# A fused attention, MLP and routed-expert kernel: a common x2 tile and two common areas, first expert fetched in the first phase, the next three behind the first gather

## The chip, the cores and the metric

The kernel runs on one core of one Trainium2 chip. TensorE is called PE here, VectorE DVE, ScalarE ACT, GpSimd POOL and SyncE SP. SP computes nothing and issues most transfers. The metric is the time of one execution on the device, in microseconds. Lower is better.

## The reference, cut to what matters

Three layers follow each other. A gated linear recurrence over 768 positions for 4 x 8 heads of 48 channels gives 3072 rows of 384 channels (x). An MLP (384 to 2048 to 384, a leaky ReLU with a learned slope) turns x into x2. Then each row is either left alone or sent to one of 8 experts:

```
skip_score = x @ w_skip
do_compute = skip_score > 0
out = x.copy()
xc = x[do_compute]
logits = xc @ w_gate
e_idx = np.argmax(logits, axis=1)
gate_w = probs[np.arange(len(xc)), e_idx]
for e in range(E):
    mask = e_idx == e
    h = np.maximum(xc[mask] @ w1[e], 0.0)
    y[mask] = gate_w[mask, None] * (h @ w2[e])
out[do_compute] = xc + y
```

Here x is the x2 of the MLP. w1 is 8 x 384 x 1024 and w2 is 8 x 1024 x 384, both float32: 1.5 MB each for one expert.

## The kernel before

The program has two phases, each a block of five hand-written instruction streams, one for each engine. Semaphores alone order them. A block ends when all five engines have come to a barrier, and the next begins there.

**Phase 1** handles the rows in eight halves of 384 rows. `step(h)` couples the attention of half h with the MLP of half h-1, so there are eight attention steps, of which seven carry an MLP, and behind the last (h = 7, the last coupled step) stands one MLP pass alone. In a step SP (`step` inside `block.sync`) goes through three chunks c of 128 rows: it loads q, k and v of the next chunk (`load_qkv`), moves decayed q and k from `qk_dec` to `kq` (`move_qk`), moves the attention's output to `xT` (`move_y`, line 359), moves the state (`move_state`, line 367), and at c = 1 calls a function `ahead`, which loads gates for a later half and does nothing in the last coupled step. At the end of each MLP, ACT copies the result from PSUM to the tile `x2` (line 687) and SP stores it twice: to `out` (line 378), as the value of rows that no expert gets, and to `x2_rows` (line 379), a scratch tensor in HBM from which phase 2 gathers. The last instruction of SP in phase 1 waits for the last of these stores.

**Phase 2** has three parts.
- *Routing.* DVE turns the logits, which lie in SBUF, into a table of slots: a slot is a group of up to 128 rows for one expert. PE multiplies the table together with matmuls (line 1274). At the end DVE copies the first slot's row numbers to `gather_at`.
- *The expert slots.* POOL gathers a slot's rows from `x2_rows` into `x_in` (line 1595, an indirect DMA). PE turns them (`turn_x`, line 1280), ACT copies the turned rows from PSUM to `xT_e` (`place_x`, line 1343), PE runs the up matmuls (line 1303), ACT and DVE make the two parts of `hT` (lines 1375, 1544), PE runs the down matmuls (line 1317), DVE adds and POOL scatters to `out` (line 1599). The next slot's gather is issued when the rows of the one before are turned and kept.
- *The expert weights.* There are four buffers for w1 (`w1_v`) and for w2 (`w2_raw`), used by experts p and p + 4. SP's `load(i, p)` issues w1 (line 1248) and w2 (line 1251) of expert 4i + p. ACT splits w2 into a high part (`split`, line 1349) and DVE into a low part (line 1514), so that PE can multiply them at its faster float format with little loss. SP issues experts 0, 1 and 2 at once, and expert 3 when the table is full, because the table's tiles lie in its buffers. Expert 4 is issued when two experts are done, and so on.

ACT's program at the beginning of phase 2, word for word:

```
            split(0, 0)
            split(0, 1)
            place_x(1)
```

After the first slot of expert p (in its program, behind the next slot's `place_x`) ACT splits expert p + 2.

Of the kernel before, what the change touches and what calls it, by code (L numbers as in the profile page):

```python
# [8 lines left out]
ALU = mybir.AluOpType  # L9
# [3 lines left out]
P = 128  # L13
BATCH, HEADS, SEQ, D = 4, 8, 768, 48
DM = HEADS * D
KT = DM // P
TOKENS = BATCH * SEQ
CH = 128
NC = 3
HT = NC * CH  # L20
HALVES = TOKENS // HT
# [9 lines left out]
FE = 1024  # L31
NFE = FE // P
LANES = EXPERTS + 1
GATE_COLS = LANES + 1
DL = DM + GATE_COLS
SLOTROWS = (TOKENS // P + EXPERTS + 1) * P
NOWHERE = 1 << 20
BODY = 4
# [47 lines left out]
def val(count):  # L86

    return count.value() if isinstance(count, Count) else count
# [24 lines left out]
def build(nc, qk, v, a, mask_in, w_in, w_pack, alpha, w_skip, w_gate, w1, w2, out, x2_rows):  # L113
    with ExitStack() as ctx:
        def sem(name):
            return ctx.enter_context(nc.semaphore(name))

        def sb(name, shape, dt=F32):
            return ctx.enter_context(nc.sbuf_tensor(name, shape, dt))

        mlp_ps = [ctx.enter_context(nc.psum_tensor(f"mlp_ps{i}", [P, 512], F32)) for i in range(2)]
        out_ps = [ctx.enter_context(nc.psum_tensor(f"out_ps{i}", [P, 512], F32)) for i in range(3)]
        att_ps = [ctx.enter_context(nc.psum_tensor(f"att_ps{i}", [P, 512], F32)) for i in range(3)]

        ident = sb("ident", [P, P])
        logits = sb("logits", [P, NT, LANES])

        phase1(nc, qk, v, a, mask_in, w_in, w_pack, alpha, w_skip, w_gate, out, x2_rows,
               mlp_ps, out_ps, att_ps, ident, logits)
        phase2(nc, w1, w2, out, x2_rows, mlp_ps, out_ps, att_ps, ident, logits)  # L130


def phase1(nc, qk, v, a, mask_in, w_in, w_pack, alpha, w_skip, w_gate, out, x2_rows,
           mlp_ps, out_ps, att_ps, ident, logits):
    with ExitStack() as ctx:
        def sem(name):
            return ctx.enter_context(nc.semaphore(name))

        def sb(name, shape, dt=F32):
            return ctx.enter_context(nc.sbuf_tensor(name, shape, dt))  # L140
# [8 lines left out]
        slope_side = sb("slope_side", [P, NF])  # L149
        tiny = sb("tiny", [P, 1])  # L150

        gates = [sb(f"gates{i}", [P, 2, NC * DM]) for i in range(2)]
        sq = sb("sq", [P, 2, NC * DM])
        norms = sb("norms", [P, NC * DM])
        inv = sb("inv", [P, NC * DM])
        f_packed = sb("f_packed", [P, KT, NC, 2])
        f_pair = sb("f_pair", [ROWS, 2, PAIRS, NC, 2])

        qk_raw = sb("qk_raw", [P, 2, KT, 2, CH])
        qk_dec = sb("qk_dec", [P, 2, KT, 2, CH])  # L160
        kq = sb("kq", [ROWS, HEADS, 2, CH])
        v_nat = sb("v_nat", [P, 2, DM])
# [10 lines left out]
        bent = sb("bent", [P, 2, HT])  # L173
        g = sb("g", [P, 3, HT])
        g_parts = sb("g_parts", [P, 4, 2, HT], F32R)
        x2 = sb("x2", [P, NC, DL])


        spare = gates[1][:, :, :].rearrange("p r x -> p (r x)")
# [46 lines left out]
        qk_loaded = [sem(f"qk_loaded{i}") for i in range(2)]  # L226
        v_loaded = [sem(f"v_loaded{i}") for i in range(2)]
        k_scaled = sem("k_scaled")
        qk_made = sem("qk_made")
# [14 lines left out]
        g_lo = sem("g_lo")  # L244
        g_used = sem("g_used")
        x2_taken = sem("x2_taken")
        x2_stored = sem("x2_stored")


        def att(h, name, c):  # L250

# [43 lines left out]
        def _(sp):  # L295
# [20 lines left out]
            def load_qkv(h, c):  # L316
                m, _ = buffer_of(h, c)
                n = chunk_no(h, c).value()
                if not isinstance(n, int):
                    sp.reg_mov(chunk_at, n)  # L320
                    n = sp.snap(chunk_at, min_val=0, max_val=HALVES * NC - 1)
                if back(h, c) and back(*back(h, c)):

                    sp.wait_ge(*filled_by("kv", back(*back(h, c))))
                if isinstance(n, int):
                    q_src, v_src = qk[n, :, :], v[n, :, :]
                else:
                    q_src = qk[bass.ds(n, 1), :, :].rearrange("n p x -> (n p) x")
                    v_src = v[bass.ds(n, 1), :, :].rearrange("n p x -> (n p) x")
                sp.dma_start(qk_raw[:, m, :, :, :].rearrange("p t w s -> p (t w s)"), q_src).then_inc(qk_loaded[m], 16)  # L330
                sp.dma_start(v_nat[:, m, :], v_src).then_inc(v_loaded[m], 16)

            def move_qk(h, c):
# [47 lines left out]
            def step(h, mlp_too, more, ahead):  # L381
                for c in range(NC):
                    if c + 1 < NC:
                        load_qkv(h, c + 1)
                        move_qk(h, c + 1)
                    elif more:
                        load_qkv(h.plus(1), 0)
                    move_y(h, c)
                    move_state(h, c)
                    if c == 1:  # L390
                        ahead()
                if more:
                    move_factors(h.plus(1))
                    move_qk(h.plus(1), 0)
                if mlp_too:
                    store_x2(h.plus(-1))
# [33 lines left out]
            with sp.Fori(0, 3) as i:  # L430
# [5 lines left out]
                    sp.nop()  # L436

                step(Half(i, 2), True, True, load_but_last)
            step(Half(0, HALVES - 1), True, False, lambda: None)
            store_x2(Half(0, HALVES - 1))  # L440
            sp.wait_ge(x2_stored, val(32 * HALVES + 1))


        @block.tensor
# [337 lines left out]
        def _(dve):  # L782
# [89 lines left out]
            def decay_qk(h, c):  # L872

                g_ = chunk_no(h, c)
                m, loads = buffer_of(h, c)
                dve.wait_ge(qk_loaded[m], loads)
                dve.wait_ge(f_inverted, val(g_ + 1))
                k_ = qk_raw[:, m, :, 1, :]
                dve.tensor_tensor(k_, k_, tiles(of_chunk(inv[:, :], c)), ALU.mult).then_inc(k_scaled, 1)
                if back(h, c):  # L880
                    dve.wait_ge(qk_moved, val(g_ * (32 * len(OP_MOVES))))
                dve.wait_ge(k_scaled, val(g_ + 1))
                for r in range(2):
                    G = tiles(of_chunk(gates[h.p][:, r, :], c)).unsqueeze(2).broadcast_to([P, KT, 2, CH])
                    last = dve.tensor_tensor(qk_dec[:, r, :, :, :], qk_raw[:, m, :, :, :], G, ALU.mult)
                last.then_inc(qk_made, 1)

            def mask_scores(h, c):
# [217 lines left out]
                               pattern=[[-1, P]], channel_multiplier=1).then_inc(consts, 1)  # L1106


def phase2(nc, w1, w2, out, x2_rows, mlp_ps, out_ps, att_ps, ident, logits):
    with ExitStack() as ctx:  # L1110
        def sem(name):
            return ctx.enter_context(nc.semaphore(name))

        def sb(name, shape, dt=F32):
            return ctx.enter_context(nc.sbuf_tensor(name, shape, dt))


        w1_v = [sb(f"w1_sb{p}", [P, KT, FE]) for p in range(BODY)]
        w2_raw = [sb(f"w2_raw{p}", [P, NFE, DM]) for p in range(BODY)]
        w2_v = [[sb(f"w2_{part}{p}", [P, NFE, DM], F32R) for part in ("hi", "lo")] for p in range(BODY)]  # L1120
        BIG = float(NOWHERE)
        NJ = NT
# [43 lines left out]
        in_row = w1_v[BODY - 1][:, :, :].rearrange("p k (t x) -> p (k t) x", x=P)  # L1166
        gather_at = sb("gather_at", [P, 1], I32)
        scatter_at = sb("scatter_at", [P, 1], I32)
        x_in = sb("x_in", [P, DM])
        x_kept_rows = sb("x_kept_rows", [P, 2, DM])  # L1170
        xT = sb("xT_e", [P, KT, P])
        hT = sb("hT", [P, 2, NFE, P], F32R)
        y = sb("y", [P, DM])

        step = sem("step")
        exp_made = sem("exp_made")
# [12 lines left out]
        tab_made = sem("tab_made")  # L1189
        first_at = sem("first_at")  # L1190
        pads_made = sem("pads_made")
        w1_loaded = [sem(f"w1_loaded{p}") for p in range(BODY)]
        w2_loaded = [sem(f"w2_loaded{p}") for p in range(BODY)]
        w2_hi = sem("w2_hi")
        w2_lo = sem("w2_lo")
        expert_done = sem("expert_done")
# [44 lines left out]
        @block.sync  # L1241
        def _(sp):
            def load(i, p):
                if i > 0:

                    sp.wait_ge(expert_done, i * BODY + p - (BODY - 3))
                    sp.wait_ge(w1_loaded[p], 16 * i)
                sp.dma_start(w1_v[p][:, :, :], expert(w1, i, p).rearrange("e (k p) f -> p (e k) f", p=P)).then_inc(w1_loaded[p], 16)  # L1248
                if i > 0:
                    sp.wait_ge(w2_lo, i * BODY + p - (BODY - 1))  # L1250
                sp.dma_start(w2_raw[p][:, :, :],
                             expert(w2, i, p).rearrange("e (f p) d -> p (e f) d", p=P)).then_inc(w2_loaded[p], 16)

            for p in range(BODY - 1):
                load(0, p)
            sp.wait_ge(table_full, 1)
            load(0, BODY - 1)
            for i in range(1, EXPERTS // BODY):
                for p in range(BODY):
                    load(i, p)  # L1260
# [315 lines left out]
        def _(pool):  # L1576
# [12 lines left out]
            pool.affine_select(out=before_pp[:, :], in_=before_pp[:, :], compare_op=ALU.is_gt, fill=0.0, base=0,  # L1589
                               pattern=[[1, P]], channel_multiplier=-1).then_inc(triangles, 1)  # L1590
            pool.memset(x_in[:, :], 0.0).then_inc(pads_made, 1)
            pool.memset(y[:, :], 0.0).then_inc(pads_made, 1)

            def gather():
                pool.indirect_dma_start(x_in[:, :], None, x2_rows, bass.IndirectOffsetOnAxis(ap=gather_at[:, 0:1], axis=0),
                                        bounds_check=TOKENS - 1, oob_is_err=False).then_inc(x_gathered, 16)
# [2 lines left out]
                pool.indirect_dma_start(out, bass.IndirectOffsetOnAxis(ap=scatter_at[:, 0:1], axis=0), y[:, :], None,  # L1599
                                        bounds_check=TOKENS - 1, oob_is_err=False).then_inc(y_stored, 16)  # L1600

            pool.wait_ge(pads_made, 2)
            pool.wait_ge(first_at, 2)
            gather()
            pool.wait_ge(slots_known, 1)
            slots_all = pool.value_load(slots_i[0:1, EXPERTS:EXPERTS + 1], min_val=0, max_val=NSLOT - 2)
            turned, kept, made = (pool.alloc_register(x) for x in ("turned", "kept", "made"))
# [92 lines left out]
```

## Time and profile before

| | |
|---|---|
| time, median of 3 runs | 968.17 us (966.34 to 971.03) |
| profiled execution | 968.83 us, span 966.9 us |
| mean granted TensorE clock | 0.922 of full speed |
| PE, DVE, ACT busy | 751.7, 699.2, 367.4 us |
| POOL busy | 51.8 us |
| loads of w1, w2 in phase 2 | 8 of 1536 KB each |
| end of phase 1 to first expert matmul | 761.6 to 805.1 us |
| expert slots | 805.1 to the end |

The span is the time from the first to the last instruction of the profiled execution. The granted clock is a share of TensorE's full speed; 1.0 stands for 2.4 GHz and 0.5 for 1.2 GHz. "Landing" is the time from the issue of a transfer to its semaphore's signal. A name such as SPq stands for an engine's sequencer, which issues transfers, waits and branches. Times in the rows count from the span's start.

### The profile page before, as it was taken

What the parts mean: (1) busy time and instruction counts of PE and PEld (TensorE: products, weight loads), DVE (VectorE), ACT (ScalarE), POOL (GpSimd) and SP (SyncE); (2) the same over time, 40 slices, a digit from 0 to 9 for tenths busy, and PEclk for the clock granted to TensorE, in tenths of its full rate; (3) what the DMA queues carried; (4) which work ended last, traced back from release to release, by engine and by line L of the source; (5) the groups of instructions that cost most, each with busy time, mean ns of one, the idle gap of its engine ahead of it and who ended that gap; (6) DMA issues with size and microseconds to landing.
All of it is one profiled execution on the core that took longest, in us unless ns stands there. A gap on an engine that the chain in (4) does not pass through costs nothing. (4 is left out here: it accounts for less than half of the span.)

```text
span 966.9 us, 16131 instructions
## 1 busy us (share of the span) xinstructions
PE 751.7 (78%) x5478; PEld 723.3 (75%) x5479; DVE 699.2 (72%) x1231; ACT 367.4 (38%) x805; POOL 51.8 (5%) x48
## 2 busy tenths in 40 slices
PE   1343456987897989889798889979999547998786
PEld 1333456987886989788688788879999447998786
DVE  6967988988999799898899989875333373434333
ACT  5452234435434534433453353334433222322221
POOL 1000000000000000000000000000000012233122
PEclk9999567999999899999999999999999857999799
DMA  6542343243342424424242352233210393324520
GB/s 188 178 152 79 93 118 90 64 130 113 80 109 62 139 65 115 126 66 133 70 118 73 100 151 63 70 113 97 57 56 1 133 357 110 126 73 163 205 82 17
DMA packets 82433, 104.74 MB, mean 108 GB/s; under 512 B 15990, under 2 KB 68384, under 8 KB 82336
## 3 DMA queue, kind: packets, MB, share of 16 engines
q1 hardware_dynamic: 80544, 99.69, 35.2%
q0 software_dynamic: 1792, 3.76, 1.2%
q8 instruction: 61, 1.00, 0.4%
q14 instruction: 36, 0.29, 0.1%
HBM read 61.04 MB, written 12.19 MB: 76 GB/s over the span
## 5 line engine op out<-in xcount | busy, mean ns | idle before, releaser
L524 PE MATMUL out_ps<-w_out_hi,g_parts 128*128 128x394 f32 x768 | 225.3, 350 | 26.3 <-DVE g_parts L933 26.3
L514 PE MATMUL mlp_ps<-xT,w_in_hi 128*128 128x384 f32 x768 | 207.1, 351 | 20.3 <-DMA xT<-y_parts 8.6
L524 PEld LDWEIGHTS out_ps<-w_out_hi,g_parts 128*128 128x128 f32 x768 | 145.9, 193 | 30.3 <-DVE g_parts L933 30.2
L514 PEld LDWEIGHTS mlp_ps<-xT,w_in_hi 128*128 128x128 f32 x768 | 140.5, 194 | 27.5 <-issue 13.5
L928 DVE SCALAR_TENSOR_TENSOR g<-mlp_ps,slope_side,bent 128x384 f32<-128x384 f32 x128 | 78.6, 615 | 83.4 <-ACT bent L666 75.3
L524 PE MATMUL out_ps<-w_out_lo,g_parts 128*128 128x394 f32 x384 | 133.8, 348 | 0.0
L514 PE MATMUL mlp_ps<-xT,w_in_lo 128*128 128x384 f32 x384 | 131.2, 342 | 0.0
L666 ACT ACTIVATE bent<-mlp_ps,bend_size 128x384 f32<-128x384 f32 x128 | 73.7, 576 | 149.5 <-PE mlp_ps L514 149.0
L1303 PE MATMUL mlp_ps<-xT_e,w_sb 128*128 128x128 f32 x624 | 79.5, 290 | 19.3 <-issue 14.1
L1303 PEld LDWEIGHTS mlp_ps<-xT_e,w_sb 128*128 128x128 f32 x624 | 77.4, 205 | 22.1 <-issue 16.9
L672 ACT ACTIVATE g_parts<-g 128x384 fp32r<-128x384 f32 x128 | 66.2, 517 | 35.4 <-DVE g L928 35.4
L468 PE MATMUL att_ps<-ident,kq 112*128 112x112 f32 x192 | 27.5, 295 | 60.8 <-DMA kq<-qk_dec 60.8
L1544 DVE SCALAR_TENSOR_TENSOR hT<-mlp_ps,hT 128x256 fp32r<-128x256 f32 x52 | 21.8, 424 | 72.8 <-ACT hT L1375 72.8
L524 PEld LDWEIGHTS out_ps<-w_out_lo,g_parts 128*128 128x128 f32 x384 | 74.1, 193 | 0.0
L514 PEld LDWEIGHTS mlp_ps<-xT,w_in_lo 128*128 128x128 f32 x384 | 74.1, 193 | 0.0
L660 ACT ACTIVATE s_t<-s_in,f_pair 112x96 f32<-112x96 f32 x192 | 53.6, 362 | 52.9 <-DVE s_in L912 34.1
L468 PEld LDWEIGHTS att_ps<-ident,kq 112*128 112x128 f32 x192 | 22.9, 160 | 65.5 <-DMA kq<-qk_dec 55.2
L933 DVE TENSOR_TENSOR g_parts<-g,g_parts 128x384 fp32r<-128x384 f32 x128 | 70.3, 549 | 0.3
L459 PE MATMUL att_ps<-kq 112*128 112x128 f32 x384 | 60.5, 320 | 5.3 <-ACT k_back L634 5.3
L798 DVE RECIPROCAL sq<-sq 128x384 f32<-128x384 f32 x24 | 61.1, 2547 | 1.2 <-ACT sq L614 1.2
L459 PEld LDWEIGHTS att_ps<-kq 112*128 112x128 f32 x384 | 57.1, 234 | 6.4 <-ACT k_back L634 6.4
L870 DVE RECIPROCAL inv<-norms 128x384 f32<-128x384 f32 x24 | 60.0, 2529 | 0.0
(150 smaller groups left out, 1082.8 us busy)
## 6 DMA issues: line engine op xcount, KB each, us to landing
kq<-qk_dec SPq DMA_DIRECT2D x96, 144.0 KB, 3.0
w_sb<-in_w SPq DMA_DIRECT2D x8, 1536.0 KB, 7.7
w_raw<-in_w SPq DMA_DIRECT2D x8, 1536.0 KB, 12.0
gates<-in_a SPq DMA_DIRECT2D x24, 384.0 KB, 4.3
qk_raw<-in_qk SPq DMA_DIRECT2D x24, 384.0 KB, 4.2
xT<-y_parts SPq DMA_DIRECT2D x48, 144.0 KB, 2.8
v_nat<-in_v SPq DMA_DIRECT2D x24, 192.0 KB, 4.0
out<-x SPq DMA_DIRECT2D x8, 576.0 KB, 3.2
```

The source lines that it names most:

```text
L459: last = pe.matmul(ps[:, n * CH:(n + 1) * CH], kq[:, slot, 1, :], kq[:, slot, 0, :], start=True, stop=True)
L468: last = pe.transpose(ps[:, n * ROWS:(n + 1) * ROWS], kq[:, PAIRS * half + n, 1, :], ident[0:ROWS, 0:ROWS])
L514: last = pe.matmul(ps[:, 0:HT], w_in_v[s][:, kk, f * P:(f + 1) * P], xT[n.p][:, kk, m, :], start=(kk == 0 and j == 0), stop=(kk == KT - 1 ...
L524: last = pe.matmul(out_ps[i][:, 0:DL], g_parts[:, f % 4, s, i * P:(i + 1) * P], w_out_v[m][:, f, :], start=(f == 0 and j == 0), stop=(f == ...
L660: last = act.activation(s_t[:, r, :, pair_, :], s_in[:, :, pair_, :], ACT.Copy, scale=f_pair[:, h.p, pair_, c, r:r + 1])
L666: act.activation(bent[:, f % 2, :], mlp_ps[f % 2][:, 0:HT], ACT.Relu, scale=bend_size[:, f:f + 1]).then_inc(bent_made, 1)
L672: act.activation(g_parts[:, f % 4, 0, :], g[:, f % 3, :], ACT.Copy).then_inc(g_hi, 1)
L798: dve.reciprocal(s1, s0).then_inc(norm_inv, 1)
L870: dve.reciprocal(of_chunk(inv[:, :], c), of_chunk(norms[:, :], c)).then_inc(f_inverted, 1)
L928: dve.scalar_tensor_tensor(out=g[:, f % 3, :], in0=mlp_ps[f % 2][:, 0:HT], scalar=slope_side[:, f:f + 1], in1=bent[:, f % 2, :], op0=ALU.m ...
L933: dve.tensor_tensor(g_parts[:, f % 4, 1, :], g[:, f % 3, :], g_parts[:, f % 4, 0, :].bitcast(F32), ALU.subtract).then_inc(g_lo, 1)
L1303: last = pe.matmul(mlp_ps[g % 2][:, (f % 2) * P:(f % 2 + 1) * P], w1_v[p][:, kk, f * P:(f + 1) * P], xT[:, kk, :], start=(kk == 0), stop=( ...
```

## The change

1. The tile `x2` becomes a part of a tile `rows` that belongs to the whole kernel. `x_in`, `x_kept_rows` and `y` of phase 2 lie in the same tile. The semaphore `x2_stored` belongs to the whole kernel too. SP no longer waits for the last stores at the end of phase 1; POOL waits for them ahead of the first gather. `x_in` lies beside x2's part, so its memset may run early; `y`'s lies in it, and its memset moves behind the first gather.
2. Two areas `arena[0]` and `arena[1]` belong to the whole kernel. In phase 1 each holds one buffer of the gates and one of raw q and k; in phase 2 the first holds w1 and the second w2 of expert 0 (and 4). SP fetches expert 0's weights in the last coupled step, at `ahead`.
3. SP issues experts 1, 2 and 3 when the first gather has landed. The wait for the full table in front of expert 3 goes, since that gather follows the table.

ACT's, PE's and DVE's programs keep their order.

```diff
+        arena = [sb(f"arena{i}", [P, KT * FE]) for i in range(2)]
+        rows = sb("rows", [P, NC * DL + DM])
+        x2_stored = sem("x2_stored")
+        first_loaded = [sem(f"first_loaded{i}") for i in range(2)]
...
-        gates = [sb(f"gates{i}", [P, 2, NC * DM]) for i in range(2)]
+        gates = [arena[i][:, 0:2 * NC * DM].rearrange("p (r x) -> p r x", r=2) for i in range(2)]
...
-        qk_raw = sb("qk_raw", [P, 2, KT, 2, CH])
+        qk_raw = [arena[i][:, 2 * NC * DM:2 * NC * DM + 2 * KT * CH].rearrange("p (t w s) -> p t w s", t=KT, w=2)
+                  for i in range(2)]
...
-        x2 = sb("x2", [P, NC, DL])
+        x2 = rows[:, 0:NC * DL].rearrange("p (i d) -> p i d", i=NC)
...
-            step(Half(0, HALVES - 1), True, False, lambda: None)
+            def fetch_first_expert():
+                sp.wait_ge(qk_made, NC * HALVES)
+                sp.dma_start(arena[0][:, :].rearrange("p (k f) -> p k f", k=KT),
+                             w1[0:1].rearrange("e (k p) f -> p (e k) f", p=P)).then_inc(first_loaded[0], 16)
+                sp.dma_start(arena[1][:, :].rearrange("p (f d) -> p f d", f=NFE),
+                             w2[0:1].rearrange("e (f p) d -> p (e f) d", p=P)).then_inc(first_loaded[1], 16)
+
+            step(Half(0, HALVES - 1), True, False, fetch_first_expert)
             store_x2(Half(0, HALVES - 1))
-            sp.wait_ge(x2_stored, val(32 * HALVES + 1))
...
-        x_in = sb("x_in", [P, DM])
-        x_kept_rows = sb("x_kept_rows", [P, 2, DM])
+        x_in = rows[:, NC * DL:NC * DL + DM]
+        x_kept_rows = rows[:, 0:2 * DM].rearrange("p (a d) -> p a d", a=2)
...
-        y = sb("y", [P, DM])
+        y = rows[:, 2 * DM:3 * DM]
...
-            for p in range(BODY - 1):
+            sp.wait_ge(x_gathered, 16)
+            for p in range(1, BODY):
                 load(0, p)
-            sp.wait_ge(table_full, 1)
-            load(0, BODY - 1)
...
-            pool.memset(y[:, :], 0.0).then_inc(pads_made, 1)
+            pool.wait_ge(x2_stored, 32 * HALVES + 1)
...
-            pool.wait_ge(pads_made, 2)
+            pool.wait_ge(pads_made, 1)
             pool.wait_ge(first_at, 2)
             gather()
+            pool.memset(y[:, :], 0.0).then_inc(pads_made, 1)
```

How SP's program reads before, from the last state moves of phase 1 to expert 3 (w_sb is a w1 buffer, w_raw a w2 buffer, in_w either weight tensor; in brackets what the row waits for):

```order
L367 DMA s_stack<-state 48x192 x3
L378 DMA out<-x 128x3x384 [waits x2_taken]
L379 DMA x_rows<-x 128x3x384
L378 DMA out<-x 128x3x384 [waits x2_taken]
L379 DMA x_rows<-x 128x3x384
L135 UNCONDITIONAL_BRANCH [waits x2_stored]
L1241 UNCONDITIONAL_BRANCH [waits barrier_Pool_Activation_PE_DVE_SP_release]
L1248 DMA w_sb<-in_w 128x3x1024
L1251 DMA w_raw<-in_w 128x8x384
```

How it reads in the changed kernel, from the second chunk's state moves of the last coupled step:

```order
L370 DMA s_stack<-state 48x192 x3
L444 DMA arena<-in_w 128x3x1024 [waits qk_made]
L446 DMA arena<-in_w 128x8x384
L362 DMA xT<-y_parts 48x6x128 [waits att_free1]
L362 DMA xT<-y_parts 48x6x128
```

And from the last stores of phase 1 on:

```order
L381 DMA out<-rows 128x3x384 [waits x2_taken]
L382 DMA x_rows<-rows 128x3x384
L139 UNCONDITIONAL_BRANCH
L1252 UNCONDITIONAL_BRANCH [waits barrier_Pool_Activation_PE_DVE_SP_release]
L1259 DMA w_sb<-in_w 128x3x1024 [waits x_gathered]
L1262 DMA w_raw<-in_w 128x8x384
L1259 DMA w_sb<-in_w 128x3x1024
```

Expert 0's two transfers moved ahead of the last chunk's moves, the wait on `x2_stored` is gone, and the first transfer of phase 2 now waits for `x_gathered`.

ACT in the changed kernel, from the end of phase 1 to its first slot (w_hi is the high part of w2):

```order
L139 UNCONDITIONAL_BRANCH
L1346 UNCONDITIONAL_BRANCH [waits barrier_Pool_Activation_PE_DVE_SP_release]
L1349 ACT_TABLE_LOAD
L1349 ACTIVATE expd<-diff 128x192 [waits diff_made]
L1359 ACTIVATE w_hi<-arena 128x3072 [waits first_loaded1]
L1359 ACTIVATE w_hi<-w_raw 128x3072 [waits w2_loaded1]
L1353 ACTIVATE xT_e<-att_ps 128x384 [waits x_turned]
```

The order is that of before; what moved is only the issue of the transfer that the second split waits for.

## Rows read from the trace of the kernel before

**Rows 1.** Waits of SP's queue: line <- releaser: total us, times, longest us.
```profile
SPq L135 <- DMA x_rows<-x: 3.7, 1, 3.7
...
SPq L135 <- PEq L135: 0.2, 1, 0.2
```

**Rows 2.** Timeline of the seam: start us, us, engine, line, instruction [idle before].
```profile
761.09 0.54 ACT L687 ACTIVATE x<-out_ps 128x384 f32<-128x384 f32 x1
...
762.06 0.49 SPq L379 DMA_DIRECT2D x_rows<-x  x1
...
766.73 0.35 DVE L1402 TENSOR_REDUCE top<-logits 128x24 f32<-128x192 f32 x1 [10.61 <-PEq L135]
```

**Rows 3.** Chain of waits, start us, us, what; first gather to ACT's copy.
```profile
794.48 8.75 DMA x_in<-x_rows,gather_at
...
803.37 0.88 PE att_ps L1280 x3
...
804.28 0.50 ACT xT_e L1343
```

**Rows 4.** Timeline of PE, first slot, turn of the next rows, and slot at 898.
```profile
805.06 7.30 PE L1303 MATMUL mlp_ps<-xT_e,w_sb 128*128 128x128 f32 x48 [0.82 <-ACT xT_e L1343]
...
812.20 0.49 PE L1280 MATMUL att_ps<-ident,x_in 128*128 128x128 f32 x3
...
898.45 8.35 PE L1303 MATMUL mlp_ps<-xT_e,w_sb 128*128 128x128 f32 x48 [6.80 <-issue]
```

**Rows 5.** Timeline of SP and PE, end of the last coupled step.
```profile
683.67 2.97 SPq L367 DMA_DIRECT2D s_stack<-state  x4
...
695.42 4.60 SPq L359 DMA_DIRECT2D xT<-y_parts  x6
...
708.98 0.51 PE L514 MATMUL mlp_ps<-xT,w_in_hi 128*128 128x384 f32 x2
```

**Rows 6.** Timeline of SP and ACT: loads of expert 0, splits of 0 and 1.
```profile
766.68 0.38 SPq L1248 DMA_DIRECT2D w_sb<-in_w  x1
...
767.11 0.48 SPq L1251 DMA_DIRECT2D w_raw<-in_w  x1
...
777.67 2.76 ACT L1349 ACTIVATE w_hi<-w_raw 128x3072 fp32r<-128x3072 f32 x1 [9.32 <-DMA w_raw<-in_w]
...
785.85 2.76 ACT L1349 ACTIVATE w_hi<-w_raw 128x3072 fp32r<-128x3072 f32 x1 [5.42 <-DMA w_raw<-in_w]
```

**Rows 7.** Landing of w2 loads (line 1251) issued at 767.11 and 868.63.
```profile
DMA to landing us min/median/max: 10.5/10.5/10.5
...
DMA to landing us min/median/max: 11.9/11.9/11.9
```

**Rows 8.** Landing of gathers (line 1595) starting 794, 824, 846, 868, 834.
```profile
DMA to landing us min/median/max: 8.8/8.8/8.8
...
DMA to landing us min/median/max: 3.1/3.1/3.1
...
DMA to landing us min/median/max: 5.3/5.3/5.3
...
DMA to landing us min/median/max: 6.2/6.2/6.2
...
DMA to landing us min/median/max: 9.2/9.2/9.2
```

**Rows 9.** Timeline of DVE's subtraction and POOL's first two gathers.
```profile
793.35 3.35 DVE L1514 TENSOR_TENSOR w_lo<-w_raw,w_hi 128x3072 fp32r<-128x3072 f32 x1
...
794.48 3.27 POOL L1595 DMA_INDIRECT x_in<-x_rows,gather_at  x1 [25.14 <-issue]
...
805.13 1.00 POOL L1595 DMA_INDIRECT x_in<-x_rows,gather_at  x1 [7.38 <-PE att_ps L1280]
```

**Rows 10.** Windows: us, busy by engine, granted clock, DMA share, GB/s.
```profile
808.00:809.00 1.00, 1.00 (x8) 1.00 (x8) 0.42 (x1) 0.38 (x1) 0.00 (x0) 0.69 0.03 1
...
904.00:905.00 1.00, 1.00 (x10) 1.00 (x10) 0.42 (x1) 0.35 (x1) 0.00 (x0) 0.91 0.00 0
```

More of the change, by code:

```diff
@@ L126, in build, with phase1 @@
         logits = sb("logits", [P, NT, LANES])
[L128 to L134, printed above, removed]
+        arena = [sb(f"arena{i}", [P, KT * FE]) for i in range(2)]
+        rows = sb("rows", [P, NC * DL + DM])
+        x2_stored = sem("x2_stored")
+        first_loaded = [sem(f"first_loaded{i}") for i in range(2)]
+        phase1(nc, qk, v, a, mask_in, w_in, w_pack, alpha, w_skip, w_gate, w1, w2, out, x2_rows,
+               mlp_ps, out_ps, att_ps, ident, logits, arena, rows, x2_stored, first_loaded)
+        phase2(nc, w1, w2, out, x2_rows, mlp_ps, out_ps, att_ps, ident, logits, arena, rows, x2_stored, first_loaded)
+def phase1(nc, qk, v, a, mask_in, w_in, w_pack, alpha, w_skip, w_gate, w1, w2, out, x2_rows,
+           mlp_ps, out_ps, att_ps, ident, logits, arena, rows, x2_stored, first_loaded):
     with ExitStack() as ctx:
@@ L246, in phase1 @@
         x2_taken = sem("x2_taken")
-        x2_stored = sem("x2_stored")
         def att(h, name, c):
@@ L329, in load_qkv @@
                     v_src = v[bass.ds(n, 1), :, :].rearrange("n p x -> (n p) x")
-                sp.dma_start(qk_raw[:, m, :, :, :].rearrange("p t w s -> p (t w s)"), q_src).then_inc(qk_loaded[m], 16)
+                sp.dma_start(qk_raw[m].rearrange("p t w s -> p (t w s)"), q_src).then_inc(qk_loaded[m], 16)
                 sp.dma_start(v_nat[:, m, :], v_src).then_inc(v_loaded[m], 16)
@@ L877, in decay_qk @@
                 dve.wait_ge(f_inverted, val(g_ + 1))
-                k_ = qk_raw[:, m, :, 1, :]
+                k_ = qk_raw[m][:, :, 1, :]
                 dve.tensor_tensor(k_, k_, tiles(of_chunk(inv[:, :], c)), ALU.mult).then_inc(k_scaled, 1)
@@ L884, in decay_qk @@
                     G = tiles(of_chunk(gates[h.p][:, r, :], c)).unsqueeze(2).broadcast_to([P, KT, 2, CH])
-                    last = dve.tensor_tensor(qk_dec[:, r, :, :, :], qk_raw[:, m, :, :, :], G, ALU.mult)
+                    last = dve.tensor_tensor(qk_dec[:, r, :, :, :], qk_raw[m][:, :, :, :], G, ALU.mult)
                 last.then_inc(qk_made, 1)
@@ L1106, in _, with phase2 @@
                                pattern=[[-1, P]], channel_multiplier=1).then_inc(consts, 1)
-def phase2(nc, w1, w2, out, x2_rows, mlp_ps, out_ps, att_ps, ident, logits):
+def phase2(nc, w1, w2, out, x2_rows, mlp_ps, out_ps, att_ps, ident, logits, arena, rows, x2_stored, first_loaded):
     with ExitStack() as ctx:
@@ L1115, in sb @@
             return ctx.enter_context(nc.sbuf_tensor(name, shape, dt))
-        w1_v = [sb(f"w1_sb{p}", [P, KT, FE]) for p in range(BODY)]
-        w2_raw = [sb(f"w2_raw{p}", [P, NFE, DM]) for p in range(BODY)]
+        w1_v = [arena[0][:, :].rearrange("p (k f) -> p k f", k=KT),
+                *(sb(f"w1_sb{p}", [P, KT, FE]) for p in range(1, BODY))]
+        w2_raw = [arena[1][:, :].rearrange("p (f d) -> p f d", f=NFE),
+                  *(sb(f"w2_raw{p}", [P, NFE, DM]) for p in range(1, BODY))]
         w2_v = [[sb(f"w2_{part}{p}", [P, NFE, DM], F32R) for part in ("hi", "lo")] for p in range(BODY)]
@@ L1191, in phase2 @@
         pads_made = sem("pads_made")
-        w1_loaded = [sem(f"w1_loaded{p}") for p in range(BODY)]
-        w2_loaded = [sem(f"w2_loaded{p}") for p in range(BODY)]
+        w1_loaded = [first_loaded[0], *(sem(f"w1_loaded{p}") for p in range(1, BODY))]
+        w2_loaded = [first_loaded[1], *(sem(f"w2_loaded{p}") for p in range(1, BODY))]
         w2_hi = sem("w2_hi")
```

## The prediction

> **What bounds the kernel now.** I read the waits of the DMA-issuing queue first, because two of the three edits move transfers there. The last rows of the first phase show a wait of 3.7 us at the block's end for the last x2_rows store, and only 0.2 us for the other engines [rows 1]. The timeline of that place gives the same: the last x2 tile is copied by 761.63, both stores are issued by 762.55, and the vector engine's first routing instruction starts at 766.73 [rows 2]. Then the chain of waits: up to the first gather at 794.48 it holds routing on DVE and PE and no transfer, so loads of expert weights bound nothing there. The gather takes 8.75 us; PE turns the rows at 803.37, ACT copies them at 804.28 [rows 3], and the first expert matmul starts at 805.06 [rows 4]. So the path through the seam is: stores, routing, gather, turn, copy, expert 0. The MLP pass before it is PE's alone.
>
> I call the start of the first expert matmul X (805.06 before). Everything behind it is driven by X: slots are chained, and each of the second four experts is loaded when earlier experts are done. So the prediction is the sum of what moves X, and of what the first slots then find.
>
> **Edit 1, no wait at the seam.** The 3.7 us of [rows 1] leave the path. The two stores' issue stays in it, and so does the barrier (762.55 + 3.7 = 766.25, to about 766.7). The wait comes back on POOL ahead of the first gather. It costs nothing there: the stores land about 766.3, and the gather starts 24 us later even after the shift. Were that cover gone, the 3.7 us would be back. Bounds: a gain of 3.7, or 0 if another engine holds the barrier; the 0.2 us row says that the others are there. I take -3.7, so the gather starts at 794.48 - 3.7 = 790.78.
>
> **Edit 2, expert 0 fetched in the last coupled step.** Two 1.5 MB transfers are issued by SP behind the state moves that end at 683.67 + 2.97 = 686.64, ahead of the xT moves at 695.42 [rows 5]. The wait that they carry (all q and k decayed) is met by then, because SP passed the same count before its last kq moves. The matching pair at 766.68 and 767.11 takes 0.9 us of issue [rows 6], and its second part lands 10.5 us after its issue [rows 7], so here about 697.6. The six xT moves behind can be late by 2 to 3 us. They are all issued by 695.42 + 4.60 = 700.0, and the last MLP pass reads them at 708.98 [rows 5]; even with a generous 5 us of flight, 4 us are left for that delay. Cost 0; were the cover gone, those 2 to 3 us would stand on PE's path. Gain 0 as well: expert 0's split was done in the shade of the routing before (ACT at 777.67 [rows 6]). Moving y's memset behind the gather is nothing: POOL is idle on both sides.
>
> **Edit 3, experts 1 to 3 behind the gather.** Two effects of opposite sign.
>
> *The gather alone on the queues.* Before, it ran beside expert 3's load, issued when the table was full, and landed after 8.8 us. Five landings compare [rows 8], in the order of the group: 8.8 for it; 3.1 (the gather at 824.53) and 5.3 (846.66) with no load in the way; 6.2 (868.47) and 9.2 (834.74) with one. The 5.3 us kind is that in which POOL's own part takes 3.2 instead of 1.0 us; it occurs while DVE's long subtraction for a weight split runs. For the first gather that is so in both kernels: DVE issues the subtraction (793.35, 3.35 us) right behind the index copies, POOL's part takes 3.27 and ends 1.05 us after it, while the second gather's takes 1.00 [rows 9]. So I take 5.2 us for 8.75: it lands at 796.0, a gain of 3.55. Bounds: 3.1 and 8.75.
>
> The Trainium skill, SBUF — State Buffer, section "Who interferes with whom", infers that a tensor_tensor on VectorE takes only the read side of the port pair shared with GpSimd and leaves descriptor generation free. By that rule the gather would land after 3.1 us and the sum would be 2.1 us lower. The trace shows 3.27 us of POOL beside exactly such an instruction, so the sum goes by the trace, and the rule's outcome is the third rival.
>
> *The new wait.* ACT runs in order, and in its program the split of expert 1's w2, which waits for that w2, stands ahead of the copy that releases the first matmul. Before, expert 1's w2 was there long ahead of the gather. Now SP issues it only when the gather has landed. Behind the split on ACT stands the copy, and behind the copy PE's whole expert part and DVE's share of it. The same pair of loads on an empty queue, with more queued behind, is in the trace: first issue at 766.68, ACT's split begins at 777.67, that is 10.99 us [rows 6]. Then the split itself, 2.76 us [rows 6], and an estimated 0.1 us for SP to wake (PE's turn follows the landing, 794.48 + 8.75 = 803.23, by 0.14 [rows 3]): 795.98 + 0.1 + 10.99 + 2.76 = 809.83 for the copy. Copy behind landing was 804.28 - 803.23 = 1.05 us and becomes 13.85: a cost of 12.80. From copy to first matmul 0.78 us, as before: X = 810.6. Bounds: 10.5 or 11.9 us of landing for the w2 transfer [rows 7], the latter for +1.4; and 0 for the whole cost if ACT weren't held.
>
> So X moves by -3.7 - 3.55 + 12.80 = **+5.55 us**.
>
> **What the first slots then find.**
> - *Clock.* Before, PE turned x at 803.37, 1.7 us ahead of X, and the granted clock left 0.50 within 808 to 809; the first slot's up matmuls took 7.30 us. At 898.45 PE came out of an idle stretch with nothing ahead of it, the clock rose about 904, and the same matmuls took 8.35 us [rows 4, 10]. In the changed kernel the turn stands 14 us ahead of X, so I take the second row: +1.05. Bounds 0 and 1.05.
> - *Second gather.* It is issued 0.07 us after X [rows 9], and PE wants it at 812.20 [rows 4], 7.14 us after X (8.2 with the slow clock). Experts 1 to 3 are 9.4 MB; at 11 us for the first 3.1 and 8.2 for each further 3.1 (ACT's second split began at 785.85, 8.18 after the first, when its w2 had come [rows 6]) they fill the queues until about 823. DVE is idle then, so it is of the 3.1 us kind, and that takes 6.2 us beside a load. Cost 0, upper bound 9.2 - 7.14 = 2.1.
> - *Experts 2 and 3.* Their w2 lands about 815 and 823. ACT wants the first of them when slot 1's turned rows are copied, 8 us after X, and the other in expert 1's first slot, some 28 us after X. Cost 0.
>
> Sum: 5.55 + 1.05 = **+6.6 us**. The profiled execution has a span of 966.9 and took 968.83 us, 1.9 more; it would be 975.4. The median of the runs is 968.17, 0.66 below the profiled one, so I forecast **974.8 us**.
>
> **Rivals.**
> 1. *The second gather waits for the held-back loads too.* Place: PE's turn in expert 0's first slot. It decides when a gather on full queues takes more than 7.1 to 8.2 us. For: 8.8 and 9.2 were seen. Against: both ran beside DVE's subtraction, the second won't. Price 2.1: 976.9 us.
> 2. *ACT isn't held; the loads are off the path* (the other side). If the gather alone released the copy, only the gains would be left: -3.7 - 3.55 = -7.25, 960.9 us. It decides if expert 1's w2 is there by the time PE has turned x. Against: such a load took over 10 us from its issue [rows 7], its issue waits for that gather, and the order of ACT's rows leaves no way round.
> 3. *The first gather is of the quick kind and the clock comes back as before.* It lands after 3.1, and there is no clock term: 5.55 - 2.1 = +3.45, 971.6 us. For: 3.1 was seen at 824.53. Against: the same DVE instruction still starts 1.1 us ahead of it.
> 4. *The seam's wait isn't lost but moves* to another engine's arrival at the barrier: 6.6 + 3.7, 978.5 us. Against: the 0.2 us row.
>
> **How the numbers follow.** Forecast 0.62, rival 1 0.12, rival 2 0.07, rival 3 0.15, rival 4 0.04. A change under 0.5% (4.8 us) can't be told from none for this kernel. Slower beyond it are the forecast, less 0.03 that comes out just under 4.8, and rivals 1 and 4: 0.75. Within: rival 3 and that 0.03: 0.18. Faster: rival 2, 0.07. The range runs from 970.5 (rival 3 and a little more) to 978.5 (the forecast with 11.9 us of landing and rival 1's price, or rival 4).
>
> **What would show it.** Right: DVE's first routing row comes about 1.4 us after ACT's last x2 copy, not 5.1; the first gather lands about 5.2 us after its start; ACT stands idle for about 39 us ahead of the second weight split, with a w2 transfer as the releaser, and its copy of xT follows that split; the first expert matmul lies about 19.8 us behind the first gather's start, against 10.6 before; from there to the end the distances are those of before within 2 us. Wrong: xT copied ahead of the second split, a gap in PE around 709, or a first gather that stays above 8 us on empty queues.

## The result, and the profile after

The changed kernel takes 974.05 us in the median of 8 runs (972.05 to 976.63); the kernel before, run beside it (8 runs), 968.16. The ratio is 1.0065, with a 95% interval of 1.0046 to 1.0084. The forecast was 974.8 us. The profiled execution has a span of 972.0 us against 966.9, so 5.1 us are to be found in the two traces.

First the waits of SP's queue in the changed kernel (engine line <- releaser: total us, times, longest), which answer to [rows 1]:

```profile
SPq L1259 <- DMA rows<-x_rows,gather_at: 33.2, 1, 33.2
...
SPq L139 <- PEq L139: 0.2, 1, 0.2
```

The row of the stores is gone, and the rest of the barrier is what it was. In its place stands one wait of 33.2 us for the first gather, at the first weight load of phase 2. SP's waiting costs nothing by itself; what is queued behind it does. The timeline of the seam (start us, us, engine, line, instruction, [idle before]), to set against [rows 2]:

```profile
761.98 0.54 ACT L696 ACTIVATE rows<-out_ps 128x384 f32<-128x384 f32 x1
...
762.96 0.49 SPq L382 DMA_DIRECT2D x_rows<-rows  x1
...
763.89 0.35 DVE L1412 TENSOR_REDUCE top<-logits 128x24 f32<-128x192 f32 x1 [6.88 <-PEq L139]
```

From the start of the last x2 copy to DVE's first routing row it was 766.73 - 761.09 = 5.64 us and is 1.91. Then the same view from the first gather on, to set against [rows 3, 4, 6, 9]:

```profile
791.66 3.25 POOL L1605 DMA_INDIRECT rows<-x_rows,gather_at  x1 [25.64 <-issue]
...
797.00 0.38 SPq L1259 DMA_DIRECT2D w_sb<-in_w  x1
...
797.12 0.88 PE L1290 MATMUL att_ps<-ident,rows 128*128 128x128 f32 x3 [7.11 <-DMA rows<-x_rows,gather_at]
...
797.44 0.48 SPq L1262 DMA_DIRECT2D w_raw<-in_w  x1
...
809.34 2.76 ACT L1359 ACTIVATE w_hi<-w_raw 128x3072 fp32r<-128x3072 f32 x1 [41.18 <-DMA w_raw<-in_w]
...
812.01 0.47 ACT L1353 ACTIVATE xT_e<-att_ps 128x384 f32<-128x384 f32 x1
...
812.71 7.29 PE L1313 MATMUL mlp_ps<-xT_e,arena 128*128 128x128 f32 x48 [14.71 <-ACT xT_e L1353]
```

Read it as an order in time: the gather lands, the rows are turned at once, and then PE has nothing to do for 14.7 us, while ACT has stood 41 us in front of one split. Its releaser is the w2 transfer that SP issued at 797.44. The copy of the turned rows is ready to go from 798 on and follows only behind that split.

Stage by stage, in us, from the rows of both traces:

| stage | before | after | difference |
|---|---|---|---|
| start to last x2 copy | 761.09 | 761.98 | +0.89 |
| last x2 copy to first routing row | 5.64 | 1.91 | -3.73 |
| routing, to start of first gather | 27.75 | 27.77 | +0.02 |
| start of gather to turn | 8.89 | 5.46 | -3.43 |
| turn to first expert matmul | 1.69 | 15.59 | +13.90 |
| first expert matmul to the end | 161.84 | 159.29 | -2.55 |
| span | 966.9 | 972.0 | +5.1 |

The first row isn't an effect of the change: SP's state moves, which stand ahead of the new fetch, start 1.0 us later already, and over the ten traces that share this first phase (the changed kernel, e1 and e3 to e10) the last x2 copy starts anywhere from 757.37 to 761.98. The end of the coupled step, to set against [rows 5]:

```profile
684.67 2.95 SPq L370 DMA_DIRECT2D s_stack<-state  x4
687.67 0.58 SPq L444 DMA_DIRECT2D arena<-in_w  x1
688.30 0.49 SPq L446 DMA_DIRECT2D arena<-in_w  x1
696.30 4.61 SPq L362 DMA_DIRECT2D xT<-y_parts  x6
```

The xT moves come 11.63 us after the start of the state moves, where it was 11.75 before, and PE goes from the last coupled matmul to the pass alone without a gap:

```profile
709.69 0.34 PE L533 MATMUL out_ps<-w_out_hi,g_parts 128*128 128x394 f32 x1
709.87 0.51 PE L523 MATMUL mlp_ps<-xT,w_in_hi 128*128 128x384 f32 x2
```

### The profile page after: what moved, and what is told of

It reads as the page before. It is cut to its first block and busy times, and to the rows that moved or that the text cites. A ratio compares the mean times of both kernels' runs of the same rounds, so it can differ in the third digit from the quotient of the medians.

```text
span 972.0 us, 16130 instructions
## 1 busy us (share of the span) xinstructions
PE 754.1 (78%) x5478; PEld 726.3 (75%) x5479; DVE 699.7 (72%) x1231; ACT 367.6 (38%) x805; POOL 51.8 (5%) x48
## 5 line engine op out<-in xcount | busy, mean ns | idle before, releaser
L1313 PE MATMUL mlp_ps<-xT_e,w_sb 128*128 128x128 f32 x480 | 59.6, 286 | 7.5 <-issue 7.1
L1313 PEld LDWEIGHTS mlp_ps<-xT_e,w_sb 128*128 128x128 f32 x480 | 58.2, 201 | 9.3 <-issue 8.4
## 6 DMA issues: line engine op xcount, KB each, us to landing
w_raw<-in_w SPq DMA_DIRECT2D x6, 1536.0 KB, 11.9
```

The costliest lines, as they stand in the source:

```text
L1313: last = pe.matmul(mlp_ps[g % 2][:, (f % 2) * P:(f % 2 + 1) * P], w1_v[p][:, kk, f * P:(f + 1) * P], xT[:, kk, :], start=(kk == 0), stop=( ...
```

## The experiments

The theory is that the whole loss is one coupling: SP issues expert 1's w2 behind the gather, and ACT's program has the split of that w2 ahead of the copy that starts expert 0. The rivals are that the held-back loads cost because they come late for their own slots or crowd the slots' gathers, and that the seam or the fetch costs. The times are medians of 5 to 12 runs, each with its ratio to the kernel before, run beside it, and the 95% interval of that ratio, unless said otherwise. Edits are shown against the changed kernel, cut to what matters.

**e1: expert 1 ahead of the gather.**

```diff
+            load(0, 1)
             sp.wait_ge(x_gathered, 16)
-            for p in range(1, BODY):
+            for p in range(2, BODY):
                 load(0, p)
```

> The changed kernel, with expert 1's load issued at the start of phase 2 and only experts 2 and 3 behind the first gather. Theory (the whole loss is ACT waiting for expert 1's w2 ahead of its copy of the turned rows): the w2 is there 25 us before the gather, the copy follows the turn, first matmul about 1.8 us behind the gather's landing; 13 to 14 us less than the changed kernel, 960.5 to 962, 0.7% below the kernel before. Rival (the held-back loads cost by crowding the slots' gathers and by arriving late for their own experts): experts 2 and 3 are still behind the gather and two of three loads still crowd it, so at most a third is won back, 969 to 972. Rival (the loss is elsewhere, in the coupled step or at the seam): 974, no change.

Measured 960.0 us, ratio to before 0.9935 (0.9908 to 0.9963): 1.3% below the changed kernel by the two ratios. Its timeline:

```profile
790.62 3.24 POOL L1606 DMA_INDIRECT rows<-x_rows,gather_at  x1 [25.64 <-issue]
...
796.07 0.87 PE L1291 MATMUL att_ps<-ident,rows 128*128 128x128 f32 x3 [7.11 <-DMA rows<-x_rows,gather_at]
...
797.70 7.22 PE L1314 MATMUL mlp_ps<-xT_e,arena 128*128 128x128 f32 x48 [0.75 <-ACT xT_e L1354]
```

Turn to first matmul is 1.63 us again. One load moved, two still held, and the whole loss is back: the first rival falls. What the two held loads do cost shows at the third gather (807.17). Expert 3's load is still under way beside it, and PE idles for 0.69 us ahead of the turn of those rows:

```profile
815.53 0.55 PE L1291 MATMUL att_ps<-ident,rows 128*128 128x128 f32 x3 [0.69 <-DMA rows<-x_rows,gather_at]
```

**e4: ACT's order.**

```diff
             split(0, 0)
-            split(0, 1)
             place_x(1)
+            split(0, 1)
```

> The changed kernel with two lines of ACT exchanged: it copies the turned rows ahead of the split of expert 1's w2. All loads stay where the change has them. Theory (the place in ACT's order is what couples the first slot to the load): the first matmul comes about 1.8 us behind the gather's landing, not 15.8, but ACT then stands in the split when the first result is ready, so the first hT comes when w2 has landed and been split, 15 us behind the landing against 19 before; PE has two groups of up matmuls done by then and the clock may have fallen again; 3 to 5 us less than the changed kernel, 969 to 971. Rival (the order on ACT doesn't matter, DVE or PE wait for the loads too): 974.

Measured 970.26 us, ratio 1.0039 (1.0015 to 1.0062), between the kernel before and the changed one. The interval overlaps that of the changed kernel (1.0046 to 1.0084), so the gain over it isn't clear by time alone; the trace carries the reading. The timeline shows the stall where it was forecast, on the other side of the copy:

```profile
793.43 0.49 ACT L1353 ACTIVATE xT_e<-att_ps 128x384 f32<-128x384 f32 x1 [29.88 <-PE att_ps L1290]
794.19 5.01 PE L1313 MATMUL mlp_ps<-xT_e,arena 128*128 128x128 f32 x24 [0.80 <-ACT xT_e L1353]
...
804.52 2.76 ACT L1359 ACTIVATE w_hi<-w_raw 128x3072 fp32r<-128x3072 f32 x1 [10.60 <-DMA w_raw<-in_w]
...
808.06 2.29 PE L1313 MATMUL mlp_ps<-xT_e,arena 128*128 128x128 f32 x9 [8.86 <-DVE hT L1554]
```

PE starts 1.7 us behind its turn (792.52 in that trace), fills both mlp_ps buffers with two groups (24 of 48 matmuls), and waits 8.86 us, because ACT stands at the split, first waiting for its w2 and then in it, and can't take them. The load is as late as before; what it stops is set by ACT's order. With e1 this shows the coupling from both sides.

**e8: w2 ahead of w1.**

```diff
             sp.wait_ge(x_gathered, 16)
-            for p in range(1, BODY):
+            sp.dma_start(w2_raw[1][:, :, :], ...).then_inc(w2_loaded[1], 16)
+            sp.dma_start(w1_v[1][:, :, :], ...).then_inc(w1_loaded[1], 16)
+            for p in range(2, BODY):
                 load(0, p)
```

> The changed kernel, with w2 of expert 1 issued ahead of its w1 behind the gather. Theory (ACT waits for exactly this w2): it lands after 8.0 us, as the first of a pair does, instead of 11.9 after an issue 0.44 later, so the first matmul comes 4.3 us earlier; w1 isn't wanted before expert 0's slots are over. 969.5 to 970, ratio to before 1.002. Rival (ACT waits for the whole pair, or a gather behind full queues is what is late): 974.

Measured 970.01 us, ratio 1.0013 (0.9995 to 1.0031). The awaited transfer and what follows it:

```profile
796.17 0.38 SPq L1266 DMA_DIRECT2D w_raw<-in_w  x1
...
804.72 2.76 ACT L1361 ACTIVATE w_hi<-w_raw 128x3072 fp32r<-128x3072 f32 x1 [37.40 <-DMA w_raw<-in_w]
...
808.09 1.22 PE L1315 MATMUL mlp_ps<-xT_e,arena 128*128 128x128 f32 x4 [10.92 <-ACT xT_e L1355]
```

From the start of the first gather to the first matmul it is 808.09 - 790.83 = 17.26 us, 3.8 less than the 21.05 of the changed kernel (812.71 - 791.66), and the time follows by 0.5%. The forecast was 4.3: ACT's split began 8.55 us after the issue of w2, not 8.0. The time goes with the arrival of exactly this w2.

**e2 and e3: the seam alone; the seam and the fetch.** In e2 the fetch in the coupled step is left out and all loads are where they were before. In e3 the fetch stays:

```diff
-            sp.wait_ge(x_gathered, 16)
-            for p in range(1, BODY):
+            for p in range(1, BODY - 1):
                 load(0, p)
+            sp.wait_ge(table_full, 1)
+            load(0, BODY - 1)
```

> The tiles of the changed kernel, no wait for the last stores at the seam, but all weight loads where they were before (0, 1, 2 at the start of phase 2, 3 with the full table) and none in the coupled step. Theory: only the 3.7 us of the seam are won, the first gather still takes 8.8 us beside expert 3's load; 964.5, ratio to before about 0.996. Rival (the stores' wait comes back elsewhere, or the new placement of tiles costs in phase 1): 968, ratio 1.000. If loads that start 3.7 us earlier beside the stores mattered, the stores would land later, and nothing would wait for them.

> As the run with the seam alone, and expert 0 fetched in the last coupled step; experts 1 and 2 at the start of phase 2, 3 with the full table. Theory: the fetch is worth nothing by itself and costs nothing; 964.5, equal to the run with the seam alone within 0.2%; first gather 8 to 9 us, because expert 3's load still starts with it. Rival (it was the rest of expert 2's load, not expert 3's, that slowed the gather): that rest is gone here, the gather takes 5.3 us and the time is 961. Rival (the fetch delays the xT moves): a gap on PE at 709 and 966 to 967.

Measured 963.79 us, ratio 0.9962 (0.9939 to 0.9984), and 962.95 us, ratio 0.9966 (0.9941 to 0.9991). The seam is worth 3.7 us by the median ratio of e2 (1.5 to 5.9 by its interval), and e2's trace has 761.61 - 759.69 = 1.92 us from the last x2 copy to the first routing row, as the changed kernel has. The fetch is worth nothing that can be measured. The first gather is slow in both. In e3 (starts of the gather and of the first matmul):

```profile
789.99 3.25 POOL L1606 DMA_INDIRECT rows<-x_rows,gather_at  x1 [25.64 <-issue]
...
800.49 0.79 PE L1314 MATMUL mlp_ps<-xT_e,arena 128*128 128x128 f32 x2 [0.75 <-ACT xT_e L1354]
```

That is 10.50 us, as before (10.58). In this trace no transfer ran from 784 to 788, so of the weight loads only expert 3's, issued at 788.36, ran beside the gather: it is that load that slows the gather.

**e5: only expert 3 held.** As e3, with the wait for the gather in place of the wait for the table:

```diff
+            for p in range(1, BODY - 1):
+                load(0, p)
             sp.wait_ge(x_gathered, 16)
-            for p in range(1, BODY):
-                load(0, p)
+            load(0, BODY - 1)
```

> The changed kernel, with experts 1 and 2 loaded at the start of phase 2 and only expert 3 behind the first gather: all three edits kept, the loads held back cut to the one that ran beside that gather before. Theory: seam 3.7 less, first gather 5.3 instead of 8.8 (expert 3's load alone slowed it: the run with the fetch and expert 3 at the full table had 10.5 us from gather to first matmul, as before), nothing waits for a weight in the first slots; 960 to 961, ratio to before 0.992 to 0.993, about 2 us less than the run with seam and fetch. Rival (what the gather wins, the second gather loses, because expert 3's load now falls on it): 963, as the run with seam and fetch.

Measured 960.76 us, ratio 0.9915 (0.9894 to 0.9935). Gather to first matmul is 7.09 us, 3.4 less than in e3:

```profile
788.23 3.25 POOL L1606 DMA_INDIRECT rows<-x_rows,gather_at  x1 [25.64 <-issue]
...
795.32 1.00 PE L1314 MATMUL mlp_ps<-xT_e,arena 128*128 128x128 f32 x3 [0.75 <-ACT xT_e L1354]
```

The held load doesn't delay the second gather enough to show: PE has no idle time ahead of the second turn. The intervals of the two ratios (0.9894 to 0.9935, and 0.9941 to 0.9991 for e3) only just miss each other; the traces set e5 clearly apart.

**e6: DVE's subtraction behind the first gather.** As e5, and:

```diff
-            split(0, 0)
             keep_x(1)
+            split(0, 0)
```

> As the run with only expert 3 held, and DVE keeps the first slot's rows ahead of its subtraction for expert 0, so that the subtraction no longer stands beside POOL's part of the first gather. Theory (the subtraction holds up POOL's descriptor work): POOL's part of the first gather takes 1.0 instead of 3.25 us, it lands after 3.1 instead of 5.3, first matmul about 4.9 us behind the gather's start instead of 7.1, 958 to 959. Rival (the Trainium skill, SBUF — State Buffer, section 'Who interferes with whom': a tensor_tensor leaves descriptor generation free; the 3.25 us are a first use of the path or chance): POOL's part stays at 3.25 and the time at 960.5. A second possibility: the subtraction falls on the second gather and delays that one instead, with a stall of PE ahead of the second turn and no gain.

Measured 957.3 us, ratio 0.9878 (0.9861 to 0.9894): the fastest version here, 1.2% below the kernel before and 1.9% below the changed one. Its interval meets that of e5 at 0.9894, so the gain over e5 rests on the trace, where it is 5.08 us from the start of the gather to the first matmul, and 7.09 in e5.

```profile
791.00 1.18 POOL L1606 DMA_INDIRECT rows<-x_rows,gather_at  x1 [25.64 <-issue]
...
794.39 0.87 PE L1291 MATMUL att_ps<-ident,rows 128*128 128x128 f32 x3 [5.05 <-DMA rows<-x_rows,gather_at]
794.62 3.35 DVE L1525 TENSOR_TENSOR w_lo<-arena,w_hi 128x3072 fp32r<-128x3072 f32 x1
...
796.08 8.39 PE L1314 MATMUL mlp_ps<-xT_e,arena 128*128 128x128 f32 x48 [0.81 <-ACT xT_e L1354]
796.15 2.70 POOL L1606 DMA_INDIRECT rows<-x_rows,gather_at  x1 [3.53 <-PE att_ps L1291]
...
804.82 0.55 PE L1291 MATMUL att_ps<-ident,rows 128*128 128x128 f32 x3 [0.34 <-DMA rows<-x_rows,gather_at]
```

POOL's part of the first gather falls from 3.25 to 1.18 us when the subtraction is gone from beside it, so the 3.25 are no cost of a first use. The second gather's part rises from 1.01 to 2.70, ending 0.88 us behind the subtraction that now stands beside it; PE waits 0.34 us for it, where e5, with expert 3's load beside the second gather too, had no wait. So here a subtraction with both inputs in SBUF does hold up POOL's part of an indirect transfer. The Trainium skill, SBUF — State Buffer, section "Who interferes with whom", infers that a tensor_tensor leaves descriptor generation free; the same section says that such an instruction, with two inputs in SBUF, contends with a GpSimd instruction that reads SBUF, and this gather takes its row numbers from there. The inference fails here; whether the reading of the row numbers is why, no run tells.

**e7, e9, e10: why the awaited w2 took 11.9 us and not 10.5.** In e7 POOL waits for expert 1's w2 ahead of the second gather. In e9 expert 3's weights are read in the place of expert 1's, so expert 1's rows get the wrong ones. In e10 nothing is queued behind the awaited w2:

```diff
 e7
+            pool.wait_ge(w2_loaded[1], 16)
             slots_all = pool.value_load(...)
 e10
             sp.wait_ge(x_gathered, 16)
-            for p in range(1, BODY):
+            load(0, 1)
+            sp.wait_ge(w2_loaded[1], 16)
+            for p in range(2, BODY):
                 load(0, p)
```

> The changed kernel, with POOL waiting for expert 1's w2 before it issues the second gather and the first scatter. In the changed kernel these two ran during that w2's transfer, which landed 11.9 us after its issue, where 10.5 was reckoned. Theory (the two crowd it): landing 10.5 and first matmul 1.4 us earlier, 19.6 us behind the first gather's start instead of 21.05. Rival (three more loads queued behind it, or HBM, make the difference): 11.9 again. No stall at the second turn is expected, since the second gather then has 7 us beside 1.4 us of split and copy, and takes 6.4.

> The changed kernel; where expert 1's weights are loaded, expert 3's are read instead, so expert 1's rows are computed with the wrong weights. Question: why the w2 behind the gather took 11.9 us from its issue in the changed kernel and 10.5 for expert 0 (10.6 for expert 3) before. If where the weights lie in HBM decides, this one lands in 10.6 as expert 3's did before, and the first matmul comes 1.3 us earlier. If what runs beside it decides (the gather after, loads queued behind), it stays at 11.7 to 11.9.

> The changed kernel with experts 2 and 3 issued only when expert 1's w2 has landed: nothing is queued behind the awaited transfer. If the loads behind crowd it, it lands in 10.5 us or less; if not, 11.7 to 11.9 again. Expert 2's w2 then lands about 20 us behind expert 1's issue and 8 us later than now, so ACT's split of it (wanted 8 us behind the first matmul) waits some 3 us and the second slot with it; time 974 to 978.

There is one execution of each, the profiled one: 974.47, 975.78 and 970.82 us. One time says little, and e10 fell outside its forecast of 974 to 978; beside e9 and e10 the kernel before took 963.97, also once. What counts here are the traces. From the issue of w2 to ACT's split it took 11.68 us in e7 (796.69 to 808.37), 11.96 in e9 (797.17 to 809.13) and 11.66 in e10 (794.46 to 806.12), against 11.90 in the changed kernel and 10.56 before (767.11 to 777.67). In e7:

```profile
796.69 0.48 SPq L1262 DMA_DIRECT2D w_raw<-in_w  x1
...
808.37 2.76 ACT L1359 ACTIVATE w_hi<-w_raw 128x3072 fp32r<-128x3072 f32 x1 [40.98 <-DMA w_raw<-in_w]
```

By one trace each, all three suspicions fall: taking away the gather and scatter beside it or the loads behind it gives 0.2 us each, and another place of the weights nothing. The w1 issued just ahead of this w2 is as late: it lands 8.0 us after its issue in the changed kernel, 8.1 in e9 and 7.9 in e10, and landed after 6.7 before, so the delay is there already in the first transfer of the pair. In e10 the next pair, expert 2's at 806.11 and 806.52, lands after 6.5 and 10.3 us, with expert 3's queued behind it. What makes the difference of some 1.3 us stays open. In e10 the stall of the second slot that I expected didn't come either: expert 2's w2 was there at 816.8, and ACT wanted it at 818.70.

## Why the prediction was right

**The seam, -3.7.** Right: -3.73 in the trace, and e2 measures it alone. The wait on POOL was hidden: routing takes 27.77 us either way.

**The fetch, 0.** Right: e2 against e3, and no gap on PE at 709.87.

**The gather, -3.55.** Right in size (-3.43 to the turn; it landed after 5.3 us) and in its two causes: expert 3's load by e3 against e5, DVE's subtraction by e6. The third rival, that the gather would be of the quick kind, fell by POOL's 3.25 us in the changed kernel.

**The new wait, +12.80.** The mechanism was right, and e1, e4 and e8 show it; the size was too small. Turn to first matmul grew by 13.90 us. The term that was mis-sized is the landing of w2: I took 10.99 us from SP's first issue to ACT's split, and it was 809.34 - 797.00 = 12.34, which is 1.35 more; the split, the copy and SP's waking took 0.25 less than I had put. The other end of the bound, 11.9 us from w2's own issue [rows 7], was the one that came. I took expert 0's pair for the value, the one on an empty queue with more queued behind it; four later pairs in the trace of before landed after 11.9 to 12.2 us, and the answer was theirs.

**The clock, +1.05.** Wrong. I had read [rows 4] as if the turn shortly ahead of X brought the clock back sooner. In the changed kernel the turn stood 15.6 us ahead and the first slot's up matmuls took 7.29 us, as before. The granted clock, one row for each microsecond:

```profile
815.00:816.00 1.00, 1.00 (x6) 1.00 (x6) 0.00 (x0) 0.33 (x1) 0.00 (x0) 0.50 1.11 414
816.00:817.00 1.00, 1.00 (x10) 1.00 (x9) 0.42 (x1) 0.05 (x1) 0.00 (x0) 0.88 1.00 397
```

It rose 3.5 us behind X, as it had 3.6 before. In e6, with the turn 1.7 us ahead as before, the same matmuls took 8.39 us, and in e10, with the turn 15 us ahead, 8.46. Over the eleven traces other than e4's (where the slot is broken in two) they took 7.02 to 8.46 us in no relation to the turn. The slot that I took the 8.35 us from scatters too: in its place, behind an idle stretch of about 7 us, the 48 matmuls took 7.00 us in e6 and 7.53 in e10, and 8.02 to 8.47 in the other ten traces. So the turn is no ground for a term; what sets the return within that scatter stays open.

**The second gather, 0.** The cost was right, the working wasn't: it isn't issued at X but when the first rows are turned and kept, at 798.89, 13.8 us ahead of X in the changed kernel. It took 6.4 us and was there 14.5 us ahead of its turn at 819.83, so the first rival had no ground. Before, both X and the second gather followed the first turn, by 1.69 and 1.76 us, and I took the 0.07 us between them for an order. Where X isn't held by the w2, crowding can reach PE: 0.69 us at the third gather in e1, beside expert 3's load, and 0.34 us at the second in e6, beside the load and the subtraction; in e5 it was nothing.

**Experts 2 and 3, 0.** Right: their w2 landed at 817.4 and 825.3, and ACT's split of expert 2 at 820.75 waited for nothing.

**The sum.** +6.6 was forecast and +5.9 measured. That the two lie so near is luck in part: the wait was 1.1 us larger, the clock's 1.05 didn't come, and what follows the first matmul was 2.55 us shorter. The signs named ahead of the run came out for the order (the copy follows the split, no gap at 709, the first gather lands after 5.3 us), with two distances larger than forecast for the reason given: ACT stood 41.2 us, not 39, and X lies 21.05 us behind the gather's start, not 19.8. One sign failed: the last stretch was to be that of before within 2 us.

The 2.55 us lie in slots near the end. Before, PE stood 2.02 us in the slot that starts at 923.05, waiting for hT, because ACT's split at 924.36 had itself waited 4.86 us for a w2; the granted clock fell to 0.50, and the next slot came 16.23 us after this one:

```profile
927.90 4.57 PE L1303 MATMUL mlp_ps<-xT_e,w_sb 128*128 128x128 f32 x24 [2.02 <-DVE hT L1544]
```

The slot in the same place of the changed kernel (932.55) had no such wait, and the next came after 11.81 us. Up to there the changed kernel was 1.85 us behind, counted from X, with two slots of 7.25 us that ran in part at the slow clock. One of them:

```profile
920.90 7.25 PE L1313 MATMUL mlp_ps<-xT_e,w_sb 128*128 128x128 f32 x48 [2.04 <-issue]
```

At the full clock the same 48 matmuls took 5.5 to 5.8 us. Over the eleven traces other than e4's the last stretch took 159.0 to 164.5 us, with the same matmuls in it. So a stage of one trace that far from the change can't be put down to it; the ratio of the timed runs carries the size.

## What to carry to other kernels

A load that is held back for one reader's sake may be awaited by another engine ahead of work that has nothing to do with it. Before you put a transfer behind an event, look through each in-order program for the first wait on it, and ask what stands behind that wait. If only one of several loads collides with something urgent, hold only that one (e5), and look at what else runs beside the urgent transfer (e6).

## What the runs showed of the hardware that was not expected

- POOL's part of an indirect gather takes 1.0 to 1.2 us alone and 2.7 to 3.6 beside DVE's 3.35 us subtraction, and ends 0.9 to 1.05 us behind it (2.70 in e6, 3.27 in [rows 9], 3.58 at 878.41 before).
- The rows of a gather that runs beside a 3 MB load reach PE 3.4 us later (8.88 us from its start in e3, 5.46 in e5), though it moves at most 0.2 MB.
- The same pair of 1.5 MB loads, with no other weight load under way, lands anywhere from 10.2 us (issued at 687.57 in e7) to 12.2 us (912.18 before) after the second's issue, mostly near 10.5 or near 11.8. A gather beside it, the loads queued behind it and the source's place, taken away one at a time (e7, e10, e9), didn't bring the low value back.
- After PE had been idle for 6.8 us or more, with at most one turn in between, the granted clock came back from 0.50 to 1.0 between 2.9 us (e7, first slot) and 6.0 us (the slot at 905.81 of the changed kernel) after work began again, in kernels with the same instructions in the slot.
